# Attention and two dense layers in one program: earlier attention units, splits in another order, and the second layer's first token pair made in tiles 3 to 7

## The reference

```python
# q, k, v: 8 batches x 8 heads x 576 tokens x 64
q_s = exp(q - max(q, over d)); q_s = q_s / sum(q_s, over d)
k_s = exp(k - max(k, over tokens)); k_s = k_s / sum(k_s, over tokens)
attn = q_s @ (k_s^T @ v)                      # -> x: 4608 tokens x 512
h = x @ w_in                                  # 512 -> 2048
x = (max(h, 0) ** 2) @ w_out                  # 2048 -> 512
xn = x / sqrt(mean(x * x) + 1e-6) * rms_g
g, val = xn @ w_gate, xn @ w_val              # 512 -> 1536 each
out = (g * sigmoid(g) * val) @ w_out2         # 1536 -> 512
```

## Time and profile before

| what | value |
|---|---|
| median of 3 runs | 1779.43 us |
| the profiled execution | 1784.51 us |
| its span, first to last instruction | 1782.8 us |
| PE busy | 1706.4 us, 96% of the span |
| DVE, ACT, POOL busy | 1066.5, 570.7, 580.3 us |
| chain that ended last | PE 84%, DVE 8%, POOL 3% |
| mean granted TensorE clock | 0.987 |

### The profile page before, as it was taken

How to read it: one execution, slowest core, us unless ns; L and a number is a source line. 1 busy time by engine, 2 the same in 40 slices (tenths; PEclk the granted TensorE clock), 3 DMA queues, 4 the chain that set the end, 5 groups by cost and what they waited for, 6 DMA issues and landing times.

```text
span 1782.8 us, 23767 instructions
## 1 busy us (share of the span) xinstructions
PE 1706.4 (96%) x8906; PEld 1503.2 (84%) x8906; DVE 1066.5 (60%) x1552; ACT 570.7 (32%) x955; POOL 580.3 (33%) x437
## 2 busy tenths in 40 slices
PE   5789999999999999999978999999999999999999
PEld 4789889988998888888866888888889998888887
DVE  7766767677656777777777674456544455322320
ACT  5433333343332323222334432233332334221220
POOL 5632333233300222222276654446555431000000
PEclk8899999999999999999999999999999999999999
DMA  6334554454364333333423222233222336344341
GB/s 191 133 128 155 162 165 146 156 169 149 120 198 158 117 120 119 122 120 119 147 90 106 82 96 99 96 122 101 78 75 91 107 102 216 122 129 131 119 141 47
DMA packets 135570, 224.85 MB, mean 126 GB/s; under 512 B 12064, under 2 KB 59680, under 8 KB 135456
## 3 DMA queue, kind: packets, MB, share of 16 engines
q1 hardware_dynamic: 135456, 223.33, 38.1%
HBM read 138.35 MB, written 84.93 MB: 125 GB/s over the span
## 4 chain that ended last, share of the span: by engine, by line
PE 84%; DVE 8%; POOL 3%; issue 2%; DMA 1%; ACT 1%; SPq 0%; DVEq 0%; ACTq 0%; POOLq 0%
PE bank L1484 15%; PE bank L1486 14%; PE bank L1485 14%; PE bank L1539 7%; PE bank L1541 7%; PE bank L1540 7%; PE bank L1611 6%; PE bank L1609 5%; PE bank L1610 5%; PE bank L1458 2%; DVE TAR L1202 2%; PE bank L1477 2%; DMA W<-in_w 1%; PE bank L1473 1%; DVE SW L1311 1%
## 5 line engine op out<-in xcount | busy, mean ns | idle before, releaser
L1484 PE MATMUL bank<-TAR,SA 128*128 128x288 f32 x896 | 292.5, 326 | 24.4 <-DVE TAR L1202 16.7
L1484 PE MATMUL bank<-TR,SW 128*128 128x460 f32 (+1 forms) x840 | 311.4, 371 | 3.3 <-DVE TR L1305 2.1
L1486 PE MATMUL bank<-TR,SW 128*128 128x460 f32 (+1 forms) x840 | 310.7, 370 | 0.0
L1485 PE MATMUL bank<-TR,SW 128*128 128x460 f32 (+1 forms) x840 | 310.5, 370 | 0.0
L1485 PE MATMUL bank<-TAR,SA 128*128 128x288 f32 x896 | 268.5, 300 | 0.0
L1486 PE MATMUL bank<-TAR,SA 128*128 128x288 f32 x896 | 268.0, 299 | 0.0
L1539 PE MATMUL bank<-GH,W 128*128 128x512 f32 x576 | 226.1, 393 | 15.5 <-DVE GH L1222 15.5
L1541 PE MATMUL bank<-GH,W 128*128 128x512 f32 x576 | 225.1, 391 | 0.0
L1540 PE MATMUL bank<-GH,W 128*128 128x512 f32 x576 | 225.1, 391 | 0.0
L1484 PEld LDWEIGHTS bank<-TAR,SA 128*128 128x128 f32 x896 | 172.5, 193 | 34.1 <-DVE TAR L1202 18.7
L1484 PEld LDWEIGHTS bank<-TR,SW 128*128 128x128 f32 x840 | 157.6, 188 | 24.7 <-issue 3.4
(11 more groups left out here) (134 smaller groups left out, 2686.0 us busy)
## 6 DMA issues: line engine op xcount, KB each, us to landing
h_scratch<-hb SPq DMA_DIRECT2D x128, 288.0 KB, 2.4
hst<-h_scratch SPq DMA_DIRECT2D x144, 256.0 KB, 2.7
AR<-a_scratch SPq DMA_DIRECT2D x54, 512.0 KB, 3.7
a_scratch<-group SPq DMA_DIRECT2D x96, 230.0 KB, 1.9
xst<-xn_scratch SPq DMA_DIRECT2D x16, 920.0 KB, 5.0
xn_scratch<-x SPq DMA_DIRECT2D x9, 1024.0 KB, 5.3
out<-ost SPq DMA_DIRECT2D x36, 256.0 KB, 4.7
kt<-in_k SPq DMA_DIRECT2D x28, 320.0 KB, 4.1
```

Source lines behind the costliest of these rows:

```text
L1484: nc.tensor.matmul(ps[:, 0:w], w_hi[:, cc], x_hi[:, c], start=opens and c == 0, stop=False, skip_group_check=True)
L1485: nc.tensor.matmul(ps[:, 0:w], w_lo[:, cc], x_hi[:, c], start=False, stop=False, skip_group_check=True)
L1486: last = nc.tensor.matmul(ps[:, 0:w], w_hi[:, cc], x_lo[:, c], start=False, stop=c == 1, skip_group_check=True)
```

## The change

Four parts, all of them in order and place; no arithmetic is added or removed.

1. **Attention units.** `UNIT_FIRST` goes from 8 to 6, so every step stands two positions earlier. Beyond that kmax moves by four more, KM, readKM, kexp and three of the loads by one more, kT by three more.
2. **Splits of layer one.** The order becomes T2, T1, B21, T3, T4, B22. The tables for ACT, DVE and POOL get new positions. In stage 1 the first weight part's sums move up on POOL, the second part's sums move behind those of T2 and T3, and ACT and DVE split all four of these token operands before the second weight part.
3. **First token pair of layer two.** It is loaded at the start of tile 3 and split at seven places from group 14 of tile 3 to group 14 of tile 7; POOL's sums for it follow `sums(2)`, `sums(3)` and `sums(4)`, cut in four pieces each. Its late splits leave groups 0 and 1 of stage 4. The third weight part's sums and split move from tile 8 and group 0 to groups 0 and 1.
4. **Norm of tile 8.** All its steps stand six groups later (`LAST_STAT = 6`), and its store follows set 2 instead of set 1.

```diff
-SPLIT_A = (B11, T1, B21, T2, T3, T4, B22)
+SPLIT_A = (B11, T2, T1, B21, T3, T4, B22)
...
-ALONE_POOL = alone_tasks(("qsub",), [(15.5, "sum", T1), (16.5, "w1", 0), (19.2, "w1", 1), (22.9, "sum", T2),
-                                     (24.4, "sum", T3), (27.0, "w1", 2)])
+ALONE_POOL = alone_tasks(("qsub",), [(12.0, "w1", 0), (15.5, "sum", T1), (22.9, "sum", T2),
+                                     (23.4, "sum", T3), (24.2, "w1", 1), (27.0, "w1", 2)])
...
-UNIT_FIRST, UNIT_PITCH = 8, 11
-UNIT_PE = [("KM", -3), ("Q0", 0), ("Q1", 1), ("KV", 2), ("X0", 6), ("X1", 7)]
+UNIT_FIRST, UNIT_PITCH = 6, 11
+UNIT_PE = [("KM", -4), ("Q0", 0), ("Q1", 1), ("KV", 2), ("X0", 6), ("X1", 7)]
...
-X_AT, XS_AT = {3: B11, 8: T2, 9: T1, 10: B21}, {4: (T1, T3, T2), 10: (T4,)}
-RAW_AT, WS_AT, S_AT = {4: 0, 7: 1, 11: 2}, {6: 0, 9: 1, 13: 2}, {7: 0, 11: 1}
+X0_LOAD = {(3, 0): 0, (3, 1): 1}
+X0_SPLIT = {(3, 14): B11, (4, 14): T2, (5, 2): T1, (5, 14): B21, (6, 2): T3, (6, 14): T4, (7, 14): B22}
+X0_SUM = {3: (T1, T3), 4: (T2,), 5: (T4,)}
+RAW_AT, WS_ALONE, S_AT = {4: 0, 7: 1, 11: 2}, 2, {7: 0, 11: 1}
...
-LATE_SUM = {0: 3, 2: 4, 3: 5}
-LATE_SPLIT = {0: 2, 1: 3, 3: 4, 4: 5}
+LATE_SUM = {0: 2, 1: 3, 2: 4, 3: 5}
+LATE_SPLIT = {1: 2, 2: 3, 3: 4, 4: 5}
+LAST_STAT = 6
...
             for u in range(NT - 1):
                 sums(u)
-            for j in range(CA):
-                for which in XS_AT.get(j, ()):
-                    x_sums(0, which, 2)
-                if j in WS_AT:
-                    w_sums(WS_AT[j])
+                for which in X0_SUM.get(u + 1, ()):
+                    x_sums(0, which, 4)
+            for m in range(WS_ALONE):
+                w_sums(m)
+            pool.wait_ge(glo_done, NR)
...
-                if q == 0:
-                    sums(NT - 1)
...
                 if q >= 1:
                     products(q - 1)
+                if q == LAST_STAT:
+                    sums(NT - 1)
```

More of the change, by code:

```diff
@@ L115, in add_batches @@
                 table.setdefault(max(0, STEPS * (b - 1) + n), []).append((what, b, i))
-add_batches(ACT_AT, "split", [(B11, 30), (T1, 50), (B21, 51), (T2, 53), (T3, 56), (T4, 58), (B22, 60)], (B11, T1, B21, T2, T3))
-add_batches(DVE_AT, "split", [(B11, 31), (T1, 51), (B21, 52), (T2, 54), (T3, 57), (T4, 59), (B22, 61)], (B11, T1, B21, T2, T3))
-add_batches(POOL_AT, "sum", [(T1, 32), (T2, 50), (T3, 52), (T4, 56)], (T1, T2, T3))
+add_batches(ACT_AT, "split", [(B11, 28), (T2, 49), (T1, 51), (B21, 52), (T3, 55), (T4, 60), (B22, 63)], (B11, T1, B21, T2, T3))
+add_batches(DVE_AT, "split", [(B11, 29), (T2, 50), (T1, 52), (B21, 53), (T3, 57), (T4, 62), (B22, 65)], (B11, T1, B21, T2, T3))
+add_batches(POOL_AT, "sum", [(T1, 30), (T2, 47), (T3, 51), (T4, 57)], (T1, T2, T3))
 for _m in range(W1_ALONE, PA):
@@ L222, in stores_of @@
     return sorted(counts.items())
-LATE_SUM = {0: 3, 2: 4, 3: 5}
-LATE_SPLIT = {0: 2, 1: 3, 3: 4, 4: 5}
+LATE_SUM = {0: 2, 1: 3, 2: 4, 3: 5}
+LATE_SPLIT = {1: 2, 2: 3, 3: 4, 4: 5}
+LAST_STAT = 6
 T_TURN = [[] for _ in range(NQ)]
 for _k in range(len(SETS)):
-    T_TURN[FIRST_Q[_k]] += [7 * _k + _i for _i in (T3, T4)]
-    T_TURN[FIRST_Q[_k] + 1] += [7 * _k + B22]
     if _k:
+        T_TURN[FIRST_Q[_k]] += [7 * _k + _i for _i in (T3, T4)]
+        T_TURN[FIRST_Q[_k] + 1] += [7 * _k + B22]
         T_TURN[LAST_Q[_k - 1] - 3] += [7 * _k + B11]
@@ L671, in _ @@
                     store_xn(u - 1)
-                if u == NT - 1 and j < 2:
-                    load_x(0, j)
+                if (u, j) in X0_LOAD:
+                    load_x(0, X0_LOAD[u, j])
                 if u == NT - 1 and j in RAW_AT:
@@ L1045, in _ @@
                     standard(u - 1)
-                if u == NT - 1:
-                    if j in X_AT:
-                        t_split(X_AT[j])
-                    if j in S_AT:
-                        s_split(S_AT[j])
+                if (u, j) in X0_SPLIT:
+                    t_split(X0_SPLIT[u, j])
+                if u == NT - 1 and j in S_AT:
+                    s_split(S_AT[j])
             def copy_p1(q):
@@ L1106, in _ @@
                 silu1(q)
-                if q == 1:
+                if q == LAST_STAT + 1:
                     squares_hi(NT - 1)
@@ L1110, in _ @@
                     silu2(q - 1)
-                if q == 3:
+                if q == LAST_STAT + 3:
                     standard(NT - 1)
@@ L1406, in _ @@
                 value2(q)
-                if q in (6, 7):
-                    recip(NT - 1, 2 * (q - 6))
-                    recip(NT - 1, 2 * (q - 6) + 1)
-                if q in (8, 9):
+                turn = q - LAST_STAT - 6
+                if turn in (0, 1):
+                    recip(NT - 1, 2 * turn)
+                    recip(NT - 1, 2 * turn + 1)
+                if turn in (2, 3):
                     for c in range(2):
-                        norm(NT - 1, 2 * (q - 8) + c)
+                        norm(NT - 1, 2 * (turn - 2) + c)
             a_split(2)
```

20 lines of the change are left out of this document (10 added, 10 removed).

## The result

The changed kernel takes 1749.2 us (median of 4 runs, 1746.8 to 1750.9), the kernel before in runs beside it 1780.4 (1779.2 to 1781.8): a ratio of 0.9824, with a 95% interval of 0.9806 to 0.9841. That is 31.2 us less; forecast were 22.1 less and 1757, with a range of 1746 to 1768. The direction, the largest term and the mechanism held; a second term was four times too small.

What follows compares the result with a forecast made beforehand. PE was taken as the bound, busy 1706.4 of 1782.8 us, with 76.4 idle and low-clock stretches at stake. Terms -19.8 - 3.8 + 1.5 = -22.1 us, from the median 1779.4 to 1757.3, range 1746 to 1768.

Steps and rivals of the forecast that it cites:

- The second layer's start: Tile 8 to group 5's B11: 23.3 us lost can go, 3.5 come back as a new wait; -19.8, between -24 and -12.
- the norm's wait: Group 8 of layer two: PE waits 3.5 us for `copy_p1` behind POOL's sums of the moved norm, between 0 and 8.
- The attention units: First layer's batches: 18.4 us of waits go, 9.8 and 4.8 come; -3.8 us, between -18 and +11.
- late splits: Start of each batch: DVE's queue delays T1's product by 0.3 us and T3's split by 0.5; +4.8 over six starts.
- Removed: Waits that go at each of six batch starts: T2's split 1.37 us, KM 1.16, a query transpose 0.35.
- KM behind X1: Third and fourth unit of seven batches: KM waits 0.7 us for ACT's X0 read, 14 places; +9.8, between 0 and 15.
- The last batch: Seventh batch start of the first layer, which has no unit: 1.15 us of waiting goes.
- The start: Kernel start: T2's 7.3 us given back at KM, +4 at the first h store, -2.8 for KM; +1.5, between -7 and +6.
- Attention clean: Rival, chance 0.15: only a third of the attention units' 14.6 new us come; term -13.5, time 1747.6.
- The last tile bound by DVE: Rival, chance 0.17: 5 us stay in the tile, or the moved norm holds 8 instead of 3.5; -10.3, 1766.8.
- the slower KM: Rival, chance 0.03: KM behind X1 waits for a full ACT queue at 14 places; at 3.8 us each +43, 1801.
- the late first pair: Rival, chance 0.02: layer two's first pair isn't ready sooner, five tiles lose what tile 8 gains; 1776 to 1780.

## Why the prediction was right, and where it was off

*The second layer's start, -19.8: right.* 20.1 by its own run. PE has no GH wait above 1 us, the clock is 1.00, and one wait for `copy_p1` comes at group 8. Inside the term, the norm's wait was set at 3.5 and costs 2.2 to 2.5. The size needed no cause, since it took the whole excess over PE's own work as removable, and that came true. The cause was too narrow: I led most of the loss back to ACT's 8.27 us behind POOL's differences. By the runs this is some 6 of the 20, by subtraction; the token splits with T4's difference are 7 to 8, and the norm's old place 6 to 7, which I had treated as something that only costs.

*The attention units, -3.8: wrong in size, and this is the step that failed.* By the traces it is -12.7 in the six batches and -3.2 in the last (-1.5 against the trace of the run with the old attention). Start and units together were forecast at -2.3 and measured at -11.4. Per batch I had 2.88 us removed, 1.40 for two KM waits and 0.80 for late splits, so 0.68 gained; measured are 2.1. The parts:

- Removed: "1.37 us for T2's split, 1.16 for KM, 0.35 for a query transpose" took the idle time shown as the price of a stop. Each stop costs about 0.26 more (0.27 for T2's split and 0.25 for KM in the rows above; the transpose's was not read), so 2.88 + 3 x 0.26 = 3.66. This is the largest part of the error, 0.78 of 1.4.
- KM behind X1: 0.7 predicted each, 1.09 / 2 = 0.55 measured. The estimate from ACT's rows was a quarter too high, and better than the 0.3 that the changed kernel's view of waits gives.
- Splits: T1's is in time, T3's is 0.48 late as shown and costs 0.73, against 0.3 + 0.5. The splits of T2, T1 and B21 at the start of a batch take 0.75 to 0.79 each; T3's takes 1.69, since it alone starts behind POOL's instruction. T1's 0.75 is what the rule quoted in the prediction gave.
- 3.66 - 1.09 - 0.73 = 1.8, and 0.3 of the 2.1 are left; the matmuls of KV, 27.2 us in the six batches before and 26.0 after, are 0.2 of them. Why they are shorter was not tried.
- The last batch: 1.15 predicted, 3.2 between the two traces. But it scatters between traces of the same code. With the old attention it took 46.1 and 47.0 us; with the new one 43.5 to 44.3 in the four traces in which PE waits 1.5 to 1.9 us for ACT's copies of h, and 44.6 to 45.9 in the four in which it waits 3.0 to 3.6. The granted clock falls for some us behind such a wait in most of the latter, but the longest of them, 45.9 (the kernel with the key maximum early), had it at 1.00 to the end of the batch, so the clock is not the cause of the scatter. The change's own part is some 2: T2's stop with its hidden part, 1.4, and a rest that is not traced.

*The start, +1.5: near by the traces, in part by luck, and nothing by the time.* The wait for T2 went from 7.3 to 2.5, and KM's from 4.9 to 14.6, given back as foreseen. The two other parts of the sum did not come, and cancelled. The wait at the stored h, 3.81 before, which I had expected to grow by 4, went, and two of 1.4 us came at 76 and 79 us. And the 2.78 for KM at 99.91, which I had expected to go, was followed by one as long, for the read of X that the next term is about:

```profile
97.90 0.32 PE L1464 MATMUL bank<-ident,kmax 128*128 128x128 f32 x1 [2.89 <-ACT xa L926]
```

With the old lists group 8 was reached at 119.3, 117.4 and 117.2, with the new at 119.7, 118.8, 121.5, 119.0 and 120.4, so +1.9 by the means; the run made for it, with 118.2 against 119.2, finds no difference in the time.

*The rivals.* "Attention clean" gave 1747.6 and is the nearest number, but for another reason: the new waits came (14 x 0.55 + 6 x 0.73 = 12.1 us of the 14.6), and what was removed was worth more. Its argument would have misled (and DVE's free time in it is 108 us, not 107). The last tile bound by DVE, the slower KM and the late first pair did not come.

## What to carry to other kernels

The idle time in front of a matmul is less than the stop costs. Measure a stop from start to start, between the same instructions where they flow and where they wait; here it is 0.2 to 0.3 us a stop beyond what is shown, which for waits of 0.3 us adds two thirds to the price. A wait that disappears at the start of a kernel says nothing, unless the slowest chain there, here POOL's weight sums up to the first stop, gets shorter. And when a crowded stage empties, ask for each of the engines in it what it did: DVE, ACT and POOL all held this one up, and the wait shown named DVE.

## What the runs showed that I had not expected

- The kernel with KM late, T3's split earlier and the sums spread is the fastest, with either start: 1734.4 and 1734.0, 15 us below the changed kernel, and its PE has no idle time from 115 to 482 us.
- One position in a table (KM, its read and its exponential) was worth 7.4 us, where the waits shown add up to 3.8 in the six batches.
- DVE's split of T3, 1.69 us, became 0.70 by starting 0.16 us ahead of POOL's instruction, which then took 1.66 instead of 1.26.
